# Building the decay turns on two engines: ScalarE takes four to six of eight heads, and the last batch's restacking DMAs leave from two queues

## Chip, core and metric

The kernel runs on one core of a Trainium2 chip. The metric is the device time of one execution in microseconds; lower is better. The core has TensorE (PE) for matmuls, VectorE (DVE), ScalarE (ACT) and GpSimd (POOL) for elementwise work, and SyncE (SP), which here only issues DMAs. ScalarE issues DMAs too, on a queue of its own (ACTq).

## What is computed

The input passes a linear attention with a complex decay, then a soft mixture of experts, then a feed-forward block. The change lies wholly in the first part:

```python
B, H, S, D = 4, 8, 768, 48
mag = np.sqrt(a_re * a_re + a_im * a_im)
scale = np.minimum(mag, 0.999) / (mag + 1e-06)
a_re_n, a_im_n = (a_re * scale, a_im * scale)
for t in range(S):
    ar, ai = (a_re_n[:, :, t, :, None], a_im_n[:, :, t, :, None])
    new_re = ar * S_re - ai * S_im
    new_im = ar * S_im + ai * S_re
    kv = np.einsum('bhd,bhe->bhde', k[:, :, t], v[:, :, t])
    S_re, S_im = (new_re + kv, new_im)
    y[:, :, t] = np.einsum('bhd,bhde->bhe', q[:, :, t], S_re)
...
x = _moe_ref(x=x, **moe_kwargs)      # soft routing over 8 experts x 4 slots, relu(x @ w1) @ w2
return _moe2_ref(x=x, **moe2_kwargs) # h = relu(x @ w_in); h * h @ w_out
```

## The kernel before

**Tiling.** Each of the 4 batches is cut into 6 chunks of 128 time steps, 24 chunks in all, numbered n = 0 to 23; c is a chunk's place in its batch. The recurrence becomes matmuls: running products of the decays (the scan) scale keys and queries, chunk scores are masked and applied to the values, and a state of 112x384 passes from chunk to chunk.

**Passes.** An outer loop p = 0 to 4 runs the scan of batch p beside the attention of batch p - 1. VectorE does most of the scan (`product_step`, `block_step`, `square_sums`, `turn_factors`) and, for a chunk, `key_query` (L934) and `weigh` (L916), `build_turn` (L946) and `apply_mask` (L955). The order on every engine is written out by hand; an engine stops at the first semaphore that isn't there.

**A chunk on its way.** `key_query` writes keys and queries into `xout`. SP's `stack` (L276) then moves them by 6 DMAs of 128 KB into `stk`, where a head's 48 real lanes lie on partitions 0 to 47 and its imaginary ones on 64 to 111. The turn is what multiplies the state between two chunks: for each head a 112x96 block in `stk`, a fixed 0/1 matrix `bm` times factors per row from `gst`. VectorE builds it for 8 heads in one instruction (L946), for all chunks but the last of a batch. TensorE's `scores(n)` (16 matmul instructions at L1180) waits for the six DMAs, the turn and the mask of the chunk before. ScalarE then copies the turned keys out of PSUM (`copy_kt`, two halves, L471), TensorE updates the state, ScalarE copies it (`copy_state`, L477) and the output of the chunk before (`copy_y`, L487; `copy_x`, L503; `copy_raw`, L494).

**Once per batch.** In the fifth chunk ("late") ScalarE squares the decays' products (`product_squares`, L430), VectorE sums them (L873) and makes the turns' factors `gd`, and SP's `stack_turns` (L286) moves these by 6 small DMAs into `gst`. ScalarE also writes the planes with a changed sign (`signs`, L461 to L464) without which VectorE can't start the next scan (L822).

**Fillers and weights.** `keep_busy` (L1166) puts matmuls without use between the others for the first 18 chunks; the last batch (chunks 18 to 23) has none, but for 20 ahead of `scores(18)`. The experts' weights come as halves of 768 KB, quarters of 384 KB (`load_half`, L371, and `load_part`, L377, both on ScalarE's queue) and wholes of 1536 KB (`load_w`, L291, SP).

Of the kernel before, what the change touches and what calls it, by code (L numbers as in the profile page):

```python
# [16 lines left out]
B, H, S, D = 4, 8, 768, 48  # L17
# [25 lines left out]
def program(nc, a_all, xq_all, v_all, phi, w1, w2, w_in, w_out, out):  # L43
    with ExitStack() as ctx:
        def sem(name):
            return ctx.enter_context(nc.semaphore(name))
# [150 lines left out]
        g_stacked = sem("g_stacked")  # L197
        a_done, masked, kt_copied = sem("a_done"), sem("masked"), sem("kt_copied")
        kv_done, s_copied, y_done = sem("kv_done"), sem("s_copied"), sem("y_done")
        m2_summed = sem("m2_summed")  # L200
        y_copied, x_done, x_copied = sem("y_copied"), sem("x_done"), sem("x_copied")
        last_y_copied = sem("last_y_copied")
        lgt_done, raw_copied, max_ready = sem("lgt_done"), sem("raw_copied"), sem("max_ready")
# [27 lines left out]

        def has_turn(n):
            return n % NC < NC - 1

        LOADED = [64 if k == 6 else 48 if k == 5 else 32 if k in EARLY + [10] else 16 for k in range(2 * NX)]
        ld_w = [sem(f"ld_w{k}") for k in range(2 * NX)]
# [15 lines left out]
        def _(sp):  # L252
# [16 lines left out]
            def stack(n):  # L269
                sp.wait_ge(kq_ready, 2 * (n + 1))  # L270
                if n >= NST:
                    sp.wait_ge(y_done, n - NST + 1)
                for c in range(2):
                    for t in range(DT):
                        k = c * R1 + t
                        sp.dma_start(stk[k:k + DT * (DL - 1) + 1:DT, n % NST, :, 0:2 * CH], xout[:, n % NOUT, c, t])\  # L276
                          .then_inc(stacked[n % NST], 16)

            def stack_turns(b):
                sp.wait_ge(chain, C_ALL * (b + 1))  # L280
                if b:
                    sp.wait_ge(rot_ready, (NC - 1) * b)
                for c in range(2):
                    for t in range(DT):
                        k = c * R1 + t
                        sp.dma_start(gst[k:k + DT * (DL - 1) + 1:DT],  # L286
                                     gd[:, c, t].rearrange("p c g -> p (c g)")).then_inc(g_stacked, 16)
# [77 lines left out]
        def _(act):  # L365

            def load_half(i):

                k, half = EARLY[i // 2], slice(i % 2 * KM * FE // 2, (i % 2 + 1) * KM * FE // 2)
                src = (w2 if k % 2 else w1)[k // 2].rearrange("p a b -> p (a b)")  # L370
                act.dma_start(wt[k][:, half], src[:, half]).then_inc(ld_w[k], 16)  # L371

            def load_part(k, i, j):
# [2 lines left out]
                src = (w2 if k % 2 else w1)[k // 2].rearrange("p a b -> p (a b)")  # L376
                act.dma_start(wt[k][:, part], src[:, part]).then_inc(ld_w[k], 16)  # L377

            def take_squares(b, t):
                act.wait_ge(ld_raw[t], 16 * (b + 1))  # L380
                if b == 0:

                    nc.scalar.activation(grid(U_ + t * PT, [1, PT]), grid(RAW + t * PT, [1, PT]), ACT.Square).then_inc(squares, 1)
                    return
                act.wait_ge(an_ready, DT * (b - 1) + t + 1)
                nc.scalar.activation(grid(U_ + t * PT, [1, PT]), grid(RAW + t * PT, [1, PT]), ACT.Square).then_inc(squares, 1)
                nc.scalar.activation(grid(V_ + t * PT, [1, PT]), grid(RAW + PF + t * PT, [1, PT]),
                                     ACT.Square).then_inc(squares, 1)
# [77 lines left out]
            def copy_kt(n, half):  # L466
                k = turns(n)
                act.wait_ge(a_done, 2 * n + half + 1)
                if k:
                    act.wait_ge(kv_done, k)  # L470
                nc.scalar.activation(kts[:, HB * half:HB * (half + 1), :], sk_ps(half, CH, KR), ACT.Copy).then_inc(kt_copied, 1)  # L471

            def copy_state(n):
                act.wait_ge(kv_done, turns(n) + 1)
# [83 lines left out]
            for p in range(B + 1):  # L558
                for c in range(NC + 2 * (p == B)):
# [7 lines left out]
                    if p == B - 1:  # L567
                        if c == 0:
                            act.wait_ge(an_ready, DT * B)
                        load_half(c)  # L570
                    if prepares:
                        if c < 2:
                            take_squares(p + 1, c)
# [14 lines left out]
                        copy_kt(n, 0)  # L588
                    if pair is not None:
                        copy_flipped(2 * pair)  # L590
                    if p < B and late:
                        product_squares(p, 0, 1)
                    if 0 <= n < NT and has_turn(n):
                        copy_kt(n, 1)
                    if p == B and c < NC:
                        if c == 0:
                            act.wait_ge(chain, C_ALL * B)
                            act.wait_ge(kq_ready, 2 * NC * (B - 1))
                            load_part(6, 3, 4)
                        if c >= 2:  # L600
                            load_half(NC + c)

                    if p == B and c == 1:
                        load_part(10, 0, 2)
# [16 lines left out]
                    if c == NC - 1 and prepares:  # L621
                        log_sums(p, 0)
                        log_sums(p, 1)
                        table()
                        exponential(p, 0, 1)
                    if 1 <= n < NT:
                        copy_y(n - 1)
                    if c == NC - 1 and prepares:
                        signs(p + 1)
                    if c == NC - 1 and p < B:  # L630
                        exponential(p, 1, NC - 1)
                    if pair is not None:
# [139 lines left out]
        def _(dve):  # L772
# [163 lines left out]
            def build_turn(n):  # L936
                b, c = divmod(n, NC)
                if c == 0:
                    dve.wait_ge(g_stacked, 96 * (b + 1))
                if n >= NST:  # L940
                    dve.wait_ge(kv_done, turns(n - NST + 1))
                o = stk[0:KS, n % NST, :, 2 * CH:].rearrange("p h (g d) -> p h g d", g=2)
                i = bass.AP(bm, 0, [list(bm[0:KS].ap[0]), [0, H], [0, 2], [1, D]])
                g = gst[0:KS, :, 2 * c:2 * c + 2]
                g = bass.AP(gst, g.offset, [list(g.ap[0]), [2 * (NC - 1), H], [1, 2], [0, D]])
# [211 lines left out]
        def _(pe):  # L1157
# [10 lines left out]
            def scores(n):  # L1168

                turn = has_turn(n)  # L1170
                cols = SK if turn else CH
                pe.wait_ge(stacked[n % NST], 96 * (n // NST + 1))
                if turn:
                    pe.wait_ge(rot_ready, turns(n) + 1)
                for half in range(2):
                    if n:
                        pe.wait_ge(masked, 2 * (n - 1) + half + 1)
                    for h in range(HB * half, HB * (half + 1)):
                        x = stk[0:KS, n % NST, h]
# [368 lines left out]
```

## Time and profile before

| | |
|---|---|
| median of 3 runs | 613.03 us (612.97 to 613.81) |
| profiled execution | 619.11 us, span 617.4 us |
| TensorE clock granted, mean | 0.941 of full speed |
| TensorE busy | 523.8 us, 85% |
| VectorE busy | 393.0 us, 64% |
| ScalarE busy | 336.5 us, 55% |
| GpSimd busy | 138.3 us, 22% |
| the chain that ended last | PE 61%, DVE 18%, DMA 7%, ACT 6%, issue 4%, SP's queue 3% |
| batch 0 to batch 3, first scores at | 75.2, 147.2, 223.1, 294.3 us |
| last scores at; feed-forward from | 344.7 us; 394 us |

Busy time is the sum of an engine's instructions; the chain follows back from the last instruction what released it. The profile page's strip of 40 slices shows TensorE busy in tenths as 1420569995989759988899999999999999999997 and VectorE as 5899998998999898893553351499433333333322: VectorE is full up to slice 18 (some 290 us), TensorE nearly full after slice 6 except in two dips, and from slice 24 on TensorE is full to the end. All that the change touches lies between 60 and 350 us.

### The profile page before, as it was taken

How to read it: one execution, taken by the hardware profiler on the slowest of the kernel's cores; microseconds unless marked ns; L12 is line 12 of the kernel's file. 1: busy time of each engine (PE TensorE's matmuls, PEld its weight loads, DVE VectorE, ACT ScalarE, POOL GpSimd, SP SyncE). 2: the span in 40 equal slices, each digit the busy share in tenths (PEclk: the TensorE clock that was granted, in tenths of full speed). 3: DMA queues.
4: the chain of work that ended last, by engine and by line, in shares of the span. 5: the costliest groups of instructions: out<-in, count | busy, mean ns of one | idle time of the engine just before them, and what ended most of it. 6: DMA issues, size and time to landing. Idle time of an engine off the chain costs nothing.

```text
span 617.4 us, 11733 instructions
## 1 busy us (share of the span) xinstructions
PE 523.8 (85%) x4572; PEld 396.8 (64%) x4572; DVE 393.0 (64%) x651; ACT 336.5 (55%) x590; POOL 138.3 (22%) x118
## 2 busy tenths in 40 slices
PE   1420569995989759988899999999999999999997
PEld 1210247774667547766688844578888888888886
DVE  5899998998998899893553351499433333333322
ACT  6865624795558923384243412676556555565653
POOL 7000000000000000000000000166655555555553
PEclk9975779997999969997898999999999999999999
DMA  7400656547767377976787999400101001010101
GB/s 272 153 1 0 180 157 134 123 99 191 212 156 149 92 166 200 213 187 142 158 214 202 389 428 427 197 1 2 53 0 53 0 1 51 2 51 2 51 1 51
DMA packets 41607, 79.59 MB, mean 129 GB/s; under 512 B 7376, under 2 KB 29008, under 8 KB 40400
## 3 DMA queue, kind: packets, MB, share of 16 engines
q1 hardware_dynamic: 39104, 67.44, 38.6%
q10 hardware_dynamic: 2448, 11.40, 5.8%
q8 instruction: 36, 0.59, 0.4%
q14 instruction: 19, 0.16, 0.1%
HBM read 55.12 MB, written 4.72 MB: 97 GB/s over the span
## 4 chain that ended last, share of the span: by engine, by line
PE 61%; DVE 18%; DMA 7%; ACT 6%; issue 4%; SPq 3%; DVEq 0%; ACTq 0%
PE ps L1477 10%; PE ps L1473 10%; PE ps L1474 10%; PE ps L1180 8%; DMA stk<-xout 5%; PE ps L1166 3%; PE ps L1447 3%; SPq L276 3%; DVE tt L838 3%; DVE big L844 2%; DVE tt L840 2%; PE ps L1223 2%; PE ps L1220 2%; DVE xout L934 2%; PE ps L1367 2%
## 5 line engine op out<-in xcount | busy, mean ns | idle before, releaser
L1145 DVE TENSOR_TENSOR qs<-rs 128x512 f32<-128x512 f32 x96 | 82.7, 862 | 118.8 <-ACT rs L707 118.8
L768 POOL TENSOR_TENSOR hlo<-qs,hhi 128x512 fp32r<-128x512 f32 x96 | 126.1, 1314 | 125.4 <-DVE qs L1145 120.2
L1180 PE MATMUL ps<-stk 112*128 112x224 f32 (+1 forms) x384 | 87.0, 388 | 29.7 <-DMA stk<-xout 29.7
L1473 PE MATMUL ps<-hhi,who 128*128 128x512 f32 x285 | 111.0, 389 | 0.0
L1474 PE MATMUL ps<-hhi,wlo 128*128 128x512 f32 x285 | 110.9, 389 | 0.0
L1180 PEld LDWEIGHTS ps<-stk 112*128 112x128 f32 x384 | 76.8, 218 | 42.0 <-DMA stk<-xout 33.7
L707 ACT ACTIVATE rs<-ps 128x512 f32<-128x512 f32 x96 | 57.4, 598 | 82.2 <-PE ps L1447 82.1
L1166 PE MATMUL ps<-ident 128*32 128x512 bf16 x256 | 71.6, 396 | 32.0 <-DVE xout L934 32.0
L1477 PE MATMUL ps<-hlo,who 128*128 128x512 f32 x285 | 80.5, 391 | 0.1
L760 POOL MEMSET sinz<- 128x768 f32 x1 | 0.7, 738 | 337.9 <-PE ps L1223 337.9
L711 ACT ACTIVATE hhi<-rs 128x512 fp32r<-128x512 f32 x96 | 60.8, 633 | 3.1
L1477 PEld LDWEIGHTS ps<-hlo,who 128*128 128x128 f32 x285 | 53.2, 188 | 12.1 <-POOL hlo L768 1.3
L1473 PEld LDWEIGHTS ps<-hhi,who 128*128 128x128 f32 x285 | 53.5, 188 | 11.2
L1474 PEld LDWEIGHTS ps<-hhi,wlo 128*128 128x128 f32 x285 | 53.5, 188 | 11.1
L1166 PEld LDWEIGHTS ps<-ident 128*32 128x32 bf16 x256 | 20.8, 98 | 55.0 <-issue 41.7
L471 ACT ACTIVATE kts<-ps 128x384 f32<-128x384 f32 x40 | 19.3, 486 | 61.6 <-PE ps L1180 61.6
L955 DVE TENSOR_TENSOR asb<-ps,mask 128x512 f32<-128x512 f32 x48 | 32.7, 687 | 30.8 <-ACT kts L471 24.3
L934 DVE TENSOR_TENSOR xout<-big,xq 128x768 f32<-128x768 f32 x48 | 45.8, 953 | 0.5
L1447 PE MATMUL ps<-cst,ust 128*128 128x512 f32 x96 | 37.4, 392 | 0.2 <-DVE ust L1127 0.2
L1223 PE MATMUL ps<-asb,vr 128*48 128x128 f32 x384 | 35.4, 272 | 0.0
L1220 PE MATMUL ps<-stk,st 112*48 112x128 f32 x320 | 31.8, 276 | 0.0
L1242 PE MATMUL ps<-xts,phs 112*32 112x128 f32 x576 | 26.4, 281 | 4.3 <-issue 4.1
(161 smaller groups left out, 809.5 us busy)
## 6 DMA issues: line engine op xcount, KB each, us to landing
stk<-xout SPq DMA_DIRECT2D x144, 128.0 KB, 3.9
wt<-in_w SPq DMA_DIRECT2D x8, 1536.0 KB, 16.8
big<-in_a_all SPq DMA_DIRECT2D x12, 768.0 KB, 5.6
xq<-in_xq SPq DMA_DIRECT2D x24, 384.0 KB, 4.6
wt<-in_w ACTq DMA_DIRECT2D x12, 768.0 KB, 5.8
vr<-in_v_all SPq DMA_DIRECT2D x24, 192.0 KB, 4.4
out<-ost SPq DMA_DIRECT2D x5, 768.0 KB, 3.5
wins<-in_w_in SPq DMA_DIRECT2D x1, 3072.0 KB, 23.1
```

The costliest lines, as they stand in the source:

```text
L707: nc.scalar.activation(rs[:, i % NQS, :], ps[:, i % 2, :], ACT.Relu).then_inc(relu_ready, 1)
L711: nc.scalar.activation(hhi[:, i % NHS, :], rs[:, i % NQS, :], ACT.Square).then_inc(hi_ready, 1)
L768: pool.tensor_tensor(hlo[:, i % NHS, :], qs[:, i % NQS, :], hhi[:, i % NHS, :].bitcast(F32), ALU.subtract).then_inc(lo_ready, 1)
L934: dve.tensor_tensor(o, e, x, ALU.mult).then_inc(kq_ready, 1)
L1145: dve.tensor_tensor(qs[:, i % NQS, :], rs[:, i % NQS, :], rs[:, i % NQS, :], ALU.mult).then_inc(sq_ready, 1)
L1166: nc.tensor.matmul(ps[P - SL:P, bank, :], idb[:, 0:SL], idle, start=True, stop=True)
L1180: last = nc.tensor.matmul(ps[:, h // 2, h % 2 * SK:h % 2 * SK + cols], x[:, 0:CH], x[:, CH:CH + cols], start=True, stop=True)
L1223: last = nc.tensor.matmul(y, vr[:, n % NV, h * D:(h + 1) * D], asb[:, n % 2, h], start=(c == 0), stop=True)
L1447: nc.tensor.matmul(ps[:, i % 2, :], ust[:, f * P:(f + 1) * P], cst[:, t * TW:(t + 1) * TW], start=True, stop=True).then_inc(g_done, 1)
L1473: nc.tensor.matmul(accs[k], wh[k], hi, start=(f == 0), stop=False)
L1474: nc.tensor.matmul(accs[k], wl[k], hi, start=False, stop=False)
L1477: last = nc.tensor.matmul(accs[k], wh[k], lo, start=False, stop=(f == F2B - 1))
```

## The change

1. **Turns.** `act_heads(n)` says how many of the 8 heads ScalarE builds: 4 for c = 1 to 3 of batches 0 and 1, 6 for c = 1 to 4 of batch 2, none for c = 0 or in batch 3. ScalarE makes two copies of 112x48 per head, each with a scale per row; half of a turn's copies stand behind `copy_kt(n - 1, 1)`, half behind `copy_y(n - 2)`. VectorE's instruction covers the other heads.
2. **Late chunk.** `copy_kt(n, 1)` now stands ahead of the second `product_squares`.
3. **Early signs.** In a batch's last chunk `signs` stands ahead of `copy_y`, not behind it.
4. **Two queues.** In batch 3 SP issues three of a chunk's six restacking DMAs, and three of `stack_turns`; ScalarE issues the rest: `stack(18)` at the batch's start, `stack(n + 1)` behind `copy_kt(n, 1)`.
5. **Weights.** `load_half` 2 to 5 go one chunk earlier; `load_part(6, 3, 4)` moves from chunk 18 to 19.

```diff
+        def act_heads(n):
+            b, c = divmod(n, NC)
+            return 0 if c == 0 or b == B - 1 or not has_turn(n) else 6 if b == B - 2 else 4 if c < 4 else 0
...
-                for c in range(2):
+                for c in range(1 if n >= NT - NC else 2):
                     for t in range(DT):
                         k = c * R1 + t
                         sp.dma_start(stk[k:k + DT * (DL - 1) + 1:DT, n % NST, :, 0:2 * CH], xout[:, n % NOUT, c, t])\
...
+            def stack(n):
+                act.wait_ge(kq_ready, 2 * (n + 1))
+                act.wait_ge(y_done, n - NST + 1)
+                for t in range(DT):
+                    k = R1 + t
+                    act.dma_start(stk[k:k + DT * (DL - 1) + 1:DT, n % NST, :, 0:2 * CH], xout[:, n % NOUT, 1, t])\
+                       .then_inc(stacked[n % NST], 16)
...
+            def build_turn(n, part):
+                b, c = divmod(n, NC)
+                count = act_heads(n) // 2
+                if count == 0:
+                    return
+                act.wait_ge(g_stacked, 96 * (b + 1))
+                if n >= NST:
+                    act.wait_ge(kv_done, turns(n - NST + 1))
+                for h in range(H - (2 - part) * count, H - (1 - part) * count):
+                    for g in range(2):
+                        o = 2 * CH + g * D
+                        last = nc.scalar.activation(stk[0:KS, n % NST, h, o:o + D], bm[0:KS, :], ACT.Copy,
+                                                    scale=gst[0:KS, h, 2 * c + g:2 * c + g + 1])
+                if part:
+                    last.then_inc(rot_act, 1)
...
-                        load_half(c)
+                        for i in ((0,), (1, 2), (3,), (4,), (5,), ())[c]:
+                            load_half(i)
+                    if p == B and c == 0:
+                        stack(n)
...
+                    if 0 <= n < NT and has_turn(n):
+                        copy_kt(n, 1)
+                    if 0 <= n < NT - 1:
+                        build_turn(n + 1, 0)
                     if p < B and late:
                         product_squares(p, 0, 1)
-                    if 0 <= n < NT and has_turn(n):
-                        copy_kt(n, 1)
...
+                    if p == B and c < NC - 1:
+                        stack(n + 1)
...
+                        signs(p + 1)
+                    if p == B - 1 and c == NC - 1:
+                        stack_turns(p)
                     if 1 <= n < NT:
                         copy_y(n - 1)
-                    if c == NC - 1 and prepares:
-                        signs(p + 1)
+                    if 0 <= n < NT - 1:
+                        build_turn(n + 1, 1)
...
+                heads = H - act_heads(n)
+                o = stk[0:KS, n % NST, 0:heads, 2 * CH:].rearrange("p h (g d) -> p h g d", g=2)
...
+                    if act_heads(n):
+                        pe.wait_ge(rot_act, act_turns(n))
```

ScalarE's order in the late chunk of batch 0 (n = 4) up to the table load; `kts` is `copy_kt`, `chain` the count of VectorE's scan. Before:

```order
L430 ACTIVATE big<-big 128x6x288 [waits chain]
L471 ACTIVATE kts<-ps 128x384 [waits kv_done,a_done]
L525 ACTIVATE lgx<-ps 128x2x32 [waits flipped]
L430 ACTIVATE big<-big 128x6x288 [waits chain]
L471 ACTIVATE kts<-ps 128x384 [waits kv_done,a_done]
L430 ACTIVATE big<-big 128x6x96 [waits chain] x2
```

With the change:

```order
L458 ACTIVATE big<-big 128x6x288 [waits chain]
L499 ACTIVATE kts<-ps 128x384 [waits kv_done,a_done]
L570 ACTIVATE lgx<-ps 128x2x32 [waits flipped]
L499 ACTIVATE kts<-ps 128x384 [waits kv_done,a_done]
L458 ACTIVATE big<-big 128x6x288 [waits chain]
L458 ACTIVATE big<-big 128x6x96 [waits chain] x2
```

The second key copy and the second large square pass have changed places.

ScalarE's order in chunk 20 of the last batch, from its key copies to the state's copy. Before:

```order
L471 ACTIVATE kts<-ps 128x384 [waits kv_done,a_done]
L525 ACTIVATE lgx<-ps 128x2x32 [waits sums_done,flipped]
L471 ACTIVATE kts<-ps 128x384 [waits kv_done,a_done]
L371 DMA wt_76<-in_w 128x1536
L487 ACTIVATE xts<-ps 128x512 [waits x_done,y_done]
L525 ACTIVATE lgx<-ps 128x2x32 [waits sums_done,flipped]
L477 ACTIVATE st<-ps 112x384 [waits y_done,kv_done]
```

With the change:

```order
L499 ACTIVATE kts<-ps 128x384 [waits kv_done,a_done]
L570 ACTIVATE lgx<-ps 128x2x32 [waits sums_done,flipped]
L499 ACTIVATE kts<-ps 128x384 [waits kv_done,a_done]
L396 DMA stk<-xout 16x8x256 [waits y_done,kq_ready]
L396 DMA stk<-xout 16x8x256 x2
L382 DMA wt_76<-in_w 128x1536
L532 ACTIVATE xts<-ps 128x512 [waits x_done,y_done]
```

Three restacking DMAs of chunk 21 now stand behind the second key copy of chunk 20 and ahead of `copy_y(19)`.

SP's order behind the last chunk but one, with the change:

```order
L286 DMA stk<-xout 16x8x256 [waits y_done,kq_ready]
L286 DMA stk<-xout 16x8x256 x2
L302 DMA wt_83<-in_w 128x3072 [waits kq_ready]
L308 DMA wt_80<-in_w 128x768
L302 DMA wt_82<-in_w 128x3072
L308 DMA wt_85<-in_w 128x1536 [waits stacked2]
```

Before, five DMAs instead of two followed the first: 3.4 MB of weights now stand three DMAs closer to SP's `stack(23)`, while the other half of that stack leaves from ScalarE.

## Rows read from the trace of the kernel before

**Rows 1.** Busy time of each engine in two stretches: batch 0's middle; chunks 19 and 20
```profile
88.00:133.00 45.00, 44.31 (x597) 33.74 (x597) 40.74 (x74) 29.02 (x51) 0.00 (x0) 0.93 0.60 142
...
305.00:325.00 20.00, 18.45 (x272) 15.72 (x272) 9.51 (x13) 7.29 (x18) 0.00 (x0) 0.91 0.95 212
```

**Rows 2.** Timeline of PE, scores of chunks 6, 8, 12, 18 to 21 and 23
```profile
147.22 5.60 PE L1180 MATMUL ps<-stk 112*128 112x224 f32 x16 [6.48 <-DMA stk<-xout]
...
171.66 3.29 PE L1180 MATMUL ps<-stk 112*128 112x224 f32 x16 [1.77 <-DMA stk<-xout]
...
223.12 5.19 PE L1180 MATMUL ps<-stk 112*128 112x224 f32 x16 [9.64 <-DMA stk<-xout]
...
294.26 3.29 PE L1180 MATMUL ps<-stk 112*128 112x224 f32 x16
...
305.21 4.98 PE L1180 MATMUL ps<-stk 112*128 112x224 f32 x16 [1.86 <-DMA stk<-xout]
314.28 3.29 PE L1180 MATMUL ps<-stk 112*128 112x224 f32 x16
325.35 4.98 PE L1180 MATMUL ps<-stk 112*128 112x224 f32 x16 [1.58 <-DMA stk<-xout]
...
344.72 2.05 PE L1180 MATMUL ps<-stk 112*128 112x128 f32 x16
```

**Rows 3.** Timeline of DVE: where it stands idle (idle us and releaser in brackets)
```profile
142.37 0.18 DVE L822 COPY a<-big 128x36 f32<-128x36 f32 x1 [1.77 <-ACT big L464]
...
200.61 0.69 DVE L955 TENSOR_TENSOR asb<-ps,mask 128x512 f32<-128x512 f32 x1 [1.32 <-ACT kts L471]
...
290.41 0.96 DVE L946 TENSOR_TENSOR stk<-bm,gst 112x768 f32<-112x768 f32 x1 [10.02 <-DMA gst<-gd]
```

**Rows 4.** Groups by line and form, 60 to 352 us: busy us, mean ns of one
```profile
L946 DVE TENSOR_TENSOR stk<-bm,gst 112x768 f32<-112x768 f32 x20 | 19.0, 952 | 10.0 <-DMA gst<-gd 10.0
L916 DVE TENSOR_TENSOR xq<-xq,big 128x384 f32<-128x384 f32 x24 | 13.2, 552 | 0.5 <-ACT big L449 0.5
L509 ACT ACTIVATE eb<-eb 32x256 f32<-32x256 f32 x11 | 5.5, 499 | 2.6 <-DVE eb L961 2.4
...
L517 ACT ACTIVATE scale_diag<-sel,rescale 96x32 f32<-96x32 f32 x10 | 3.2, 321 | 0.3
```

**Rows 5.** Timeline of ACT: batch ends, a late chunk, key copy of chunk 20
```profile
137.60 0.60 ACT L487 ACTIVATE xts<-ps 128x512 f32<-128x512 f32 x1 [0.67 <-PE ps L1223]
138.09 0.52 ACT L461 ACTIVATE big<-big 128x384 f32<-128x384 f32 x1
...
198.51 1.64 ACT L430 ACTIVATE big<-big 128x1728 f32<-128x1728 f32 x1
200.05 0.47 ACT L471 ACTIVATE kts<-ps 128x384 f32<-128x384 f32 x1
...
290.76 0.27 ACT L494 ACTIVATE eb<-ps 96x128 f32<-96x128 f32 x1
...
317.94 0.48 ACT L471 ACTIVATE kts<-ps 128x384 f32<-128x384 f32 x1
```

**Rows 6.** The chain that ended last: start, us, what
```profile
215.80 7.28 DMA stk<-xout
...
280.70 9.69 DMA gst<-gd
```

**Rows 7.** Queues of ACT and SP: start of issue, us for all, count
```profile
214.75 0.34 ACTq L371 DMA_DIRECT2D wt<-in_w  x1
...
321.56 17.16 SPq L276 DMA_DIRECT2D stk<-xout  x12
338.76 0.60 SPq L291 DMA_DIRECT2D wt<-in_w  x1
```

**Rows 8.** DMA landing: the tile `gst`, and the page's group of stk<-xout
```profile
DMA to landing us min/median/max: 1.8/1.8/9.7
...
stk<-xout SPq DMA_DIRECT2D x144, 128.0 KB, 3.9
```

More of the change, by code:

```diff
@@ L199, in program @@
         kv_done, s_copied, y_done = sem("kv_done"), sem("s_copied"), sem("y_done")
-        m2_summed = sem("m2_summed")
+        m2_summed, rot_act = sem("m2_summed"), sem("rot_act")
         y_copied, x_done, x_copied = sem("y_copied"), sem("x_done"), sem("x_copied")
@@ L233, in has_turn, with act_turns @@
             return n % NC < NC - 1
+        def act_heads(n):
+            b, c = divmod(n, NC)
+            return 0 if c == 0 or b == B - 1 or not has_turn(n) else 6 if b == B - 2 else 4 if c < 4 else 0
+        def act_turns(n):
+            return sum(act_heads(k) > 0 for k in range(n + 1))
         LOADED = [64 if k == 6 else 48 if k == 5 else 32 if k in EARLY + [10] else 16 for k in range(2 * NX)]
@@ L282, in stack_turns @@
                     sp.wait_ge(rot_ready, (NC - 1) * b)
-                for c in range(2):
+                    sp.wait_ge(rot_act, act_turns(NC * b - 1))
+                for c in range(1 if b == B - 1 else 2):
                     for t in range(DT):
@@ L377, in load_part, with stack_turns @@
                 act.dma_start(wt[k][:, part], src[:, part]).then_inc(ld_w[k], 16)
+            def stack(n):
[5 more added lines that the diff above has]
+                       .then_inc(stacked[n % NST], 16)
+            def stack_turns(b):
+                act.wait_ge(chain, C_ALL * (b + 1))
+                act.wait_ge(rot_ready, (NC - 1) * b)
+                act.wait_ge(rot_act, act_turns(NC * b - 1))
+                for t in range(DT):
+                    k = R1 + t
+                    act.dma_start(gst[k:k + DT * (DL - 1) + 1:DT], gd[:, 1, t].rearrange("p c g -> p (c g)")).then_inc(g_stacked, 16)
             def take_squares(b, t):
@@ L590, in _ @@
                         copy_flipped(2 * pair)
+                    if 0 <= n < NT and has_turn(n):
+                        copy_kt(n, 1)
+                    if 0 <= n < NT - 1:
+                        build_turn(n + 1, 0)
                     if p < B and late:
                         product_squares(p, 0, 1)
-                    if 0 <= n < NT and has_turn(n):
-                        copy_kt(n, 1)
[L595 to L601, printed above, removed]
+                    if p == B and c < NC - 1:
+                        stack(n + 1)
+                    if p == B and c == 1:
+                        act.wait_ge(chain, C_ALL * B)
+                        act.wait_ge(kq_ready, 2 * NC * (B - 1))
+                        load_part(6, 3, 4)
+                    if p == B and 2 <= c < NC:
+                        load_half(NC + c)
                     if p == B and c == 1:
@@ L941, in build_turn @@
                     dve.wait_ge(kv_done, turns(n - NST + 1))
-                o = stk[0:KS, n % NST, :, 2 * CH:].rearrange("p h (g d) -> p h g d", g=2)
-                i = bass.AP(bm, 0, [list(bm[0:KS].ap[0]), [0, H], [0, 2], [1, D]])
+                heads = H - act_heads(n)
+                o = stk[0:KS, n % NST, 0:heads, 2 * CH:].rearrange("p h (g d) -> p h g d", g=2)
+                i = bass.AP(bm, 0, [list(bm[0:KS].ap[0]), [0, heads], [0, 2], [1, D]])
                 g = gst[0:KS, :, 2 * c:2 * c + 2]
-                g = bass.AP(gst, g.offset, [list(g.ap[0]), [2 * (NC - 1), H], [1, 2], [0, D]])
+                g = bass.AP(gst, g.offset, [list(g.ap[0]), [2 * (NC - 1), heads], [1, 2], [0, D]])
                 dve.tensor_tensor(o, i, g, ALU.mult).then_inc(rot_ready, 1)
```

## The prediction, made before the changed kernel was run

> **What bounds the kernel now.** I read the busy times by stretch first. From 88 to 133 us TensorE is busy 44.3 of 45.0 us: there a chunk costs what TensorE's own list costs, fillers included, and time saved on VectorE buys nothing. In chunks 19 and 20 the DMA engines are 95% taken [rows 1]. Then the scores on TensorE's timeline, since every chunk starts with them. Where they waited, they waited for the restacked keys: 6.48 us at chunk 6, 1.77 at chunk 8, 9.64 at chunk 12, 1.86 at 19, 1.58 at 21 [rows 2]. Those waits are VectorE's lateness (it makes the keys) plus the DMAs' time. VectorE itself is full in these stretches and stood idle for three releasers that the change touches: the sign planes (1.77 us), ScalarE's second key copy (1.32), the turn factors' DMA (10.02) [rows 3]. The last batch takes 344.72 - 294.26 = 50.46 us for five steps. Everything behind it (experts, feed-forward) is not edited and moves as a block.
>
> **The change part by part.** All sums are against the profiled execution (619.11 us; span 617.4); the median of the three runs is 613.03, 6.1 us less, and I take the difference over unchanged. About 0.2%, 1.2 us, is what a measurement of this kernel can tell from no change.
>
> *Smaller turns on VectorE.* 8 heads (768 columns) take 952 ns, and 384 columns of a like instruction 552 ns [rows 4], so a column costs 1.04 ns. Four heads fewer save 0.40 us (six turns), six fewer 0.60 us (four turns): 4.8 us of VectorE in all. In batch 0 and the middle of batch 2 TensorE sets the pace: nothing. In batch 1 turns 7 and 8 stand ahead of the keys of chunks 8 and 9, which were late: 0.8 us by chunk 9.
>
> *The copies on ScalarE.* 6 x 8 + 4 x 12 = 96 copies of 48 columns with a scale per row. The trace has no such form. With a per-row operand, 32 columns take 321 ns and 256 take 499 [rows 4]: 334 ns for 48. ScalarE's starts follow each other 0.11 us sooner than a duration (137.60 + 0.60 against 138.09) [rows 5], so 0.23 us each; 22 us in all. Bounds: 0.21 (as 32 columns) and 0.39 (as 256). Their cover is ScalarE's waits for TensorE ahead of `copy_y` and `copy_state`: it is busy 29.0 of 45.0 us there [rows 1], so 3.7 us a chunk are idle for 1.9 us of copies. It is thin in chunks 1 and 7, where squares stand there too: I charge 0.35 us in batch 0 and 0.7 in batch 1, with 0 and 3 as bounds over all. Per head VectorE pays 0.10 us and ScalarE 0.46. The Trainium skill ("ScalarE: Activation LUTs", Rules for kernel authors) says to multiply on VectorE, not ScalarE. By that rule alone the trade of 4.8 us for 22 would lose; by the idle time it costs about 1.
>
> *Second key copy first.* In the late chunk the large square pass (1.54 us from start to start) stood ahead of it [rows 5]. VectorE waited 1.32 us for the copy [rows 3], masked for 0.69 and only then summed the squares. Now the mask is done while the pass ends, and the sums start with its end: 0.6 us, in batches 0 and 1. In batch 2 the mask stands behind the sums, which get the pass 0.4 us later: -0.4 of the gain there.
>
> *Early signs.* They stood behind `copy_y`, which waited 0.67 us and took 0.49 [rows 5]; VectorE waited 1.77 us for the last of them [rows 3]. Ahead of it they end 1.2 us sooner, in batches 1 and 2. Price: `copy_y` comes behind 4.2 us of signs, 3.8 us later than before in batch 1 and 2.0 in batch 2, and TensorE's transposes with it. The waits of 6.48 and 9.64 us that follow [rows 2] hide that.
>
> So at chunk 6: 0.6 - 0.35 = 0.3 us earlier. VectorE's next scan: 0.9 (it then waits 1.2 us, not 1.77). Chunk 9: 0.9 + 0.8, less a little of ScalarE's copies, is 1.6. The keys of chunk 12: 1.6 + 0.6 = 2.2.
>
> *Chunk 12.* Its last restacking DMA took 7.28 us to land [rows 6] against a median of 3.9 [rows 8]: half 0 of the weights left at 214.75 [rows 7], in the middle of the six. That half stands behind `copy_raw(10)`, hence behind logits that wait for the delayed `copy_y`. So it leaves near 214.6 still, while the six leave 2.2 us sooner and should land in about 4.5: 2.8 more. Chunk 12 is 5.0 us earlier (bounds 2.2 and 7.0, the latter with the clock kept up, below). In batch 2 VectorE is only 2.8 us ahead, 3.4 after the turn of 13, and chunk 14 waits for it a little: 4.5 are left, and 4.1 at chunk 17.
>
> *Turn factors of batch 3.* The last of six DMAs of 5 KB took 9.69 us [rows 6], where the common one takes 1.8 [rows 8], with half 5 of the weights issued half a microsecond behind it. Half 5 now goes a chunk earlier. ScalarE's three leave only behind the logits of chunk 15, near 277.5, and should land near 281, not 290.4. This takes 9 us from VectorE's wait of 10.02; but chunk 18 was ready at 294.26 only through TensorE's own list (20 fillers), so it frees no more than the lateness of chunk 19 (1.86).
>
> *Two queues.* SP needs 3.8 us for six issues, over 0.6 each (twelve took 17 us with a wait between) [rows 7]. Half of that is saved only if ScalarE's three leave as early. They don't: they stand behind `copy_kt(n - 1, 1)`, 3.68 us after the scores' start (317.94 against 314.28) [rows 2, 5], though the keys were long ready. Scores to scores is then 3.68 + 2 x 0.64 + 3.9 = 8.9 us at least. TensorE's own list needs about 9.3 us in even chunks and 7.4 to 8.3 in odd ones (9.07 from 305.21, less 1.7 for the slow start). For chunk 18 they stand behind `copy_raw(16)`, at 290.76 [rows 5] less 4.1: with 1.28 for the issues and 3.9 they land at 291.8, or some 0.5 sooner, as an issue leaves while an earlier copy still runs; TensorE would be ready at 290.2. So chunk 18 starts near 291.4, 2.8 us earlier than before. For chunk 23 they meet the weights: SP's 3.4 MB (from 338.76 [rows 7]) leave 2 us closer to its keys and ahead of ScalarE's three. The nearest row is the small DMA caught by a half: 9.69 us. I take 7 to land, so 12 us for that step; bounds 9.4 and 13. Sum of the five steps: 9.2 + 9.2 + 9.9 + 9.6 + 12 = 49.9, against 50.46: 0.5 earlier. The clock (below) is as likely to cost 0.6 once more as not, and I take the two as even.
>
> Forecast: 2.8 us earlier at the end of the attention: 613.0 - 2.8 = **610.2 us**.
>
> **The rivals.**
>
> *A. The clock stays up.* Chunks 6, 12, 19 and 21 take 5 us or more for scores that take 3.29 elsewhere; chunk 8 doesn't, after 1.77 us idle [rows 2]. The long ones fall in stretches at the lower level (1.2 of 2.4 GHz). With the late transposes TensorE is idle 6.48 - 3.8 - 0.3 = 2.4 us ahead of chunk 6 and 9.64 - 2.0 - 5.0 = 2.6 ahead of 12. If the clock holds, each gives 1.8 us, 19 another 1.7: with the 2.8 some 8 us, **605**. Against it: after 1.58 and 1.86 us idle it fell.
>
> *B. ScalarE's queue sets the last batch's pace: slower.* If its three land in 6.3 us, as under weights, not 3.9, each of five steps is 3.68 + 1.28 + 6.3 = 11.3 us; five are 56.3, 5.8 more than before, chunk 18 loses 2.4 of its 2.8: 613.0 - 0.4 + 5.8 = 618.4; with two of the five so, 615. It decides from a landing of 5.1 us on, where a step costs the 10.1 of before. For it: DMA is 95% taken [rows 1], and idle TensorE lowers the clock, which delays the key copy by 1.3. Against: the weights stand behind the three on the same queue. The skill ("DMA: Bandwidth & Descriptors", Queues, rings and completion order) says that a completion lands only after all earlier writes of that DMA engine, across queues, so splitting does not shield a stack from SP's 3.4 MB. The 9.69 us row agrees. The same page (Issuing engines are not separate DMA queues) allows a second queue nothing but the issue time.
>
> *C. Given back.* The gains of batches 1 and 2 come, but chunk 12's keys still take 7.3 us to land: 2.2 us are left there, 0.9 behind chunk 18's wait, and a last step of 13 us makes the five 50.9 and takes 0.4 more: 0.5 left, **612.5**, no change. It decides if half 0 leaves as early as the stack does.
>
> **How the numbers follow.** Forecast 0.46, its range 608 to 611.5; A 0.22; B 0.16; C 0.16. Faster by over 0.2% (below 611.8): the forecast, A and a little of C, 0.69. Within 0.2%: 0.16. Slower: 0.15. For 8 in 10 the range runs from A, 604.5, to two bad steps of B, 615.
>
> **What would show it.** Right: scores of 12 near 218 after a landing of 4 to 5 us; VectorE's wait for the signs near 1.2; turn factors landed near 281; ACT copies of 0.33 us; steps of 9 to 10 us in the last batch with waits of 0 to 2 on restacking DMAs, and the longest before 23. Wrong: a gap ahead of chunk 8 or 12 as before, TensorE waiting for `rot_act`, ScalarE's `copy_state` late in batch 2, or a last batch over 52 us.

## The result, and the profile after

The changed kernel takes **629.88 us** (median of 6 runs, 624.09 to 631.25) against 613.42 for the kernel before beside it: a ratio of 1.0249 [1.0201, 1.0298]. The prediction was 610.2 us, faster; its range ended at 615. The profiled execution is an ordinary one (629.77 us, span 628.0). Ratios, here and below, stand with their 95% intervals and leave out the few runs that fell in a slower state of the chip; the medians keep them.

Timeline of PE of the changed kernel, the scores of chunks 6, 8, 12, 14, 18, 22 and 23 (start us, us, instruction, in brackets the idle time before it and its releaser), as [rows 2]:

```profile
145.97 5.04 PE L1237 MATMUL ps<-stk 112*128 112x224 f32 x16 [1.12 <-DMA stk<-xout]
...
172.91 3.54 PE L1237 MATMUL ps<-stk 112*128 112x224 f32 x16
...
220.54 5.30 PE L1237 MATMUL ps<-stk 112*128 112x224 f32 x16 [0.55 <-DMA stk<-xout]
...
247.09 4.97 PE L1237 MATMUL ps<-stk 112*128 112x224 f32 x16 [3.83 <-DMA stk<-xout]
...
297.99 3.29 PE L1237 MATMUL ps<-stk 112*128 112x224 f32 x16 [1.00 <-DMA stk<-xout]
...
334.72 3.29 PE L1237 MATMUL ps<-stk 112*128 112x224 f32 x16
...
354.03 3.78 PE L1237 MATMUL ps<-stk 112*128 112x128 f32 x16 [8.82 <-DMA stk<-xout]
```

Chunk 12 is 2.6 us earlier than in [rows 2] (223.12); by chunk 18 that is lost (297.99 against 294.26); and chunk 23 starts 19.31 us after chunk 22, where the kernel before took 9.42 (344.72 in [rows 2] less the start of chunk 22):

```profile
335.30 3.29 PE L1180 MATMUL ps<-stk 112*128 112x224 f32 x16
```

TensorE stands idle for 8.82 us for one DMA. The chain of waits of the changed kernel names it in its last row (the first is a wait for chunk 14's stack, taken up at the end), and the answer for `stk<-xout` on ScalarE's queue gives the landing:

```profile
238.36 8.69 DMA stk<-xout
...
339.00 1.19 ACTq L396
340.23 13.76 DMA stk<-xout
```
```profile
DMA to landing us min/median/max: 2.7/3.5/13.8
```

The queues of the changed kernel at that place (start of issue, us for all, count), as [rows 7]:

```profile
331.31 0.61 ACTq L382 DMA_DIRECT2D wt<-in_w  x1
331.95 0.48 ACTq L388 DMA_DIRECT2D wt<-in_w  x1
338.40 2.45 ACTq L396 DMA_DIRECT2D stk<-xout  x3
...
334.91 0.62 SPq L302 DMA_DIRECT2D wt<-in_w  x1
335.57 0.59 SPq L308 DMA_DIRECT2D wt<-in_w  x1
336.20 0.78 SPq L302 DMA_DIRECT2D wt<-in_w  x1
354.00 0.33 SPq L308 DMA_DIRECT2D wt<-in_w  x1
```

SP has done its own half of stack 23 and issues 3.4 MB of weights from 334.91 on; ScalarE's half follows from 338.40 and lands at 353.99. SP's own half, issued 0.7 to 1.9 us ahead of the weights, took 6.9 to 7.9 us to land; ScalarE's three took 8.9, 12.9 and 13.8. From 340 to 354 us the DMA engines are full:

```profile
340.00:354.00 14.00, 5.03 (x102) 3.14 (x99) 0.42 (x1) 3.36 (x9) 0.00 (x0) 0.77 1.01 330
```

The last three numbers are TensorE's granted clock (0.77), the DMA engines' busy share (all of it) and 330 GB/s.

The turns and the signs stand in the trace as priced (groups by form; timeline of DVE, as [rows 3]):

```profile
L513 ACT ACTIVATE stk<-bm,gst 112x48 f32<-112x48 f32 x96 | 23.5, 325 | 0.0
...
L1001 DVE TENSOR_TENSOR stk<-bm,gst 112x384 f32<-112x384 f32 x6 | 3.3, 553 | 0.0
L1001 DVE TENSOR_TENSOR stk<-bm,gst 112x192 f32<-112x192 f32 x4 | 1.4, 352 | 0.0
```
```profile
139.80 0.18 DVE L876 COPY a<-big 128x36 f32<-128x36 f32 x1 [1.16 <-ACT big L492]
...
214.93 0.18 DVE L876 COPY a<-big 128x36 f32<-128x36 f32 x1 [1.27 <-ACT big L492]
...
290.49 0.96 DVE L1001 TENSOR_TENSOR stk<-bm,gst 112x768 f32<-112x768 f32 x1 [6.02 <-DMA gst<-gd]
```

The copies take 325 ns (334 expected) and 23.5 us in all (22), the turns 553 and 352 ns, and VectorE waits 1.2 us for the signs instead of 1.8. VectorE's busy time falls from 393.0 to 388.2 us, the 4.8 us of the sum.

The two first profiles differ by 10.7 us and the medians by 16.5, since the profiled execution of before was 6 us above its own median. The first experiment asks where those 6 us lay.

### The profile page after: what moved, and what is told of

It reads as the page before. It is cut to its first block, busy times and chain, and to the rows that moved or that the text cites. A ratio compares the mean times of both kernels' runs of the same rounds, so it can differ in the third digit from the quotient of the medians.

```text
span 628.0 us, 11862 instructions
## 1 busy us (share of the span) xinstructions
PE 528.5 (84%) x4572; PEld 397.0 (63%) x4572; DVE 388.2 (62%) x651; ACT 357.1 (57%) x686; POOL 138.2 (22%) x118
## 4 chain that ended last, share of the span: by engine, by line
PE 60%; DVE 14%; ACT 10%; DMA 8%; issue 4%; SPq 2%; ACTq 1%; DVEq 0%
PE ps L1534 10%; PE ps L1530 10%; PE ps L1531 10%; PE ps L1237 8%; DMA stk<-xout 6%; PE ps L1221 3%; PE ps L1504 3%; DMA big<-in_a_all 3%; DVE tt L892 2%; DVE big L898 2%; DVE tt L894 2%; PE ps L1299 2%; SPq L286 2%; PE ps L1277 2%; PE ps L1424 2%
## 5 line engine op out<-in xcount | busy, mean ns | idle before, releaser
L1237 PE MATMUL ps<-stk 112*128 112x224 f32 (+1 forms) x384 | 83.5, 377 | 24.0 <-DMA stk<-xout 24.0
L1221 PE MATMUL ps<-ident 128*32 128x512 bf16 x256 | 75.9, 415 | 31.4 <-DVE xout L988 31.4
L1237 PEld LDWEIGHTS ps<-stk 112*128 112x128 f32 x384 | 74.1, 212 | 36.2 <-DMA stk<-xout 28.5
L1534 PEld LDWEIGHTS ps<-hlo,who 128*128 128x128 f32 x285 | 53.2, 188 | 12.1 <-POOL hlo L822 1.4
L1299 PE MATMUL ps<-xts,phs 112*32 112x128 f32 x576 | 28.7, 297 | 5.5 <-issue 5.5
## 6 DMA issues: line engine op xcount, KB each, us to landing
wins<-in_w_in SPq DMA_DIRECT2D x1, 3072.0 KB, 16.8
```

What stands on the lines that cost most here:

```text
L1221: nc.tensor.matmul(ps[P - SL:P, bank, :], idb[:, 0:SL], idle, start=True, stop=True)
L1534: last = nc.tensor.matmul(accs[k], wh[k], lo, start=False, stop=(f == F2B - 1))
```

## The experiments

"Step 22 to 23" is from the scores of chunk 22 to those of 23, in each run's own profile. All ratios are to the kernel before, run beside it on the same chip. Its median there was 611.3 to 613.4 us, so medians of different rows can be compared to some 2 us only. Each chunk's start is from one execution. In short:

| kernel | median us | ratio | chunk 12 at | 18 at | 18 to 22 | 22 to 23 |
|---|---|---|---|---|---|---|
| before, profile shown ahead | 613.03 | 1 | 223.1 | 294.3 | 41.0 | 9.4 |
| before again | 613.41 | 1.0013 [0.9985, 1.0040] | 221.8 | 293.1 | 34.6 | 9.4 |
| the change | 629.88 | 1.0249 [1.0201, 1.0298] | 220.5 | 298.0 | 36.7 | 19.3 |
| its stack 23 on SP | 616.88 | 1.0057 [1.0016, 1.0098] | 217.4 | 294.8 | 36.2 | 9.8 |
| its last batch on one queue | 612.33 | 0.9963 [0.9924, 1.0002] | 217.3 | 294.3 | 34.4 | 9.4 |
| its SP weights held back | 621.61 | 1.0141 [1.0076, 1.0206] | 216.3 | 295.9 | 37.2 | 9.9 |
| one queue, old halves | 608.75 | 0.9960 [0.9944, 0.9976] | 217.2 | 288.2 | 35.8 | 9.4 |
| key order and signs | 609.48 | 0.9971 [0.9948, 0.9995] | 217.9 | 288.8 | 37.7 | 9.4 |
| two queues alone | 628.66 | 1.0278 [1.0241, 1.0315] | 222.4 | 294.5 | 39.4 | 20.1 |
| turns alone | 612.82 | 1.0021 [1.0001, 1.0040] | 223.4 | 293.5 | 39.4 | 9.4 |
| two queues, issued early | 620.24 | 1.0120 [1.0090, 1.0150] | 221.2 | 293.3 | 34.4 | 17.1 |
| signs alone | 608.75 | 0.9942 [0.9914, 0.9969] | 216.5 | 286.4 | 40.5 | 9.4 |
| key order alone | 612.03 | 1.0003 [0.9978, 1.0029] | 221.7 | 293.2 | 37.3 | 9.4 |
| change, old halves, early issue | 618.41 | 1.0095 [1.0071, 1.0120] | 217.9 | 289.3 | 35.0 | 17.9 |
| stack 23 alone on two queues | 623.34 | 1.0179 [1.0139, 1.0218] | 223.4 | 294.8 | 34.2 | 17.9 |
| signs, five stacks early | 609.25 | 0.9953 [0.9925, 0.9980] | 221.7 | 293.8 | 34.5 | 9.4 |

### The kernel before again

> The kernel before, unchanged, for a second profiled execution. The first one took 619.11 us where the median of its runs is 613.4, so the two profiles differ by 10.7 us and the medians by 16.5. If the first profiled execution was an unlucky one, a new one takes 612 to 615 us, and its chunks must start earlier somewhere by 4 to 7 us in all: the place of that difference is what the comparison of the two first profiles cannot show. If profiling itself costs the kernel before 5 us, the new one takes 618 to 620 again. Timed, it must be within 0.2% of the kernel before (ratio 0.998 to 1.002); what it differs is the noise of all that follows.

Measured: 611.31 us profiled, so the first profiled execution was the unlucky one. Its chunks 18 and 23 on the timeline of PE:

```profile
293.06 3.10 PE L1180 MATMUL ps<-stk 112*128 112x224 f32 x15
...
327.64 3.29 PE L1180 MATMUL ps<-stk 112*128 112x224 f32 x16
337.06 2.05 PE L1180 MATMUL ps<-stk 112*128 112x128 f32 x16
```

Chunk 18 starts 1.2 us earlier than in [rows 2], chunk 23 7.7 us earlier: the last batch's five steps take 44.0 us, not 50.46. The waits of 1.86 and 1.58 us at chunks 19 and 21 and the low clock behind them were that execution's. VectorE's wait for the turn factors is 5.99 us here, not 10.02, and it ends at 286.3, 4.2 us sooner than in the change: the 6.02 of the change shows no gain. Over the kernels with one queue in the table, 18 to 22 takes 34.2 to 41.0 us; this stretch falls out differently from execution to execution.

### Stack 23: another queue, or the bulk beside it?

```diff
-                for c in range(1 if n >= NT - NC else 2):
+                for c in range(1 if NT - NC <= n < NT - 1 else 2):
...
-                    if p == B and c < NC - 1:
+                    if p == B and c < NC - 2:
                         stack(n + 1)
```
(SP also waits for the stacks of all three buffers ahead of `load_part(10, 2, 4)`.)

> The change, but all six transfers of the last key stack, that of chunk 23, are on SP's queue, ahead of SP's 3.4 MB of weights; ScalarE keeps its halves of chunks 18 to 22 and of the turn factors. Theory T1 (SP's bulk takes the DMA engines from a small stack on the other queue), T2 (ScalarE's own bulk stands ahead of it in its queue) and T3 (ScalarE only issues it late, behind a key copy) all expect the landing to go back from 13.8 us to 4 to 6 us, the scores of chunk 23 to start near 345 us instead of 354.0, and 629.9 less 8 to 9.5 us, so 620.5 to 622. If the stack is not what costs, the time stays within 2 us of 629.9.

Measured: 616.88 us, below the 620.5 to 622 expected, and step 9.8: stack 23 is worth 13.0 us of the change by the medians, 1.9% or 11.8 us by the ratios. Three theories had one expectation here; the next run parts them. It moves SP's wait for stack 23 ahead of `load_w(8)`, and leaves ScalarE as it is in the change.

> The change, with SP's 3.4 MB of weights (three transfers issued at 334.9 to 337.0 us) held back until the stack of chunk 23 has landed; ScalarE's queue is as in the change. T1 (SP's bulk takes the DMA engines): ScalarE's half of stack 23 lands 4 to 7 us after its issue at 340.2, the scores of chunk 23 start at 345 to 347, and the time falls by 6 to 9 us to 621 to 624, unless the weights that come later cost some of it again. T2 (ScalarE's own 1.15 to 1.5 MB ahead of it in its queue): the landing stays at 11 to 14 us and the time at 628 to 632 or above. T3 (late issue alone): landing 4 us after the issue in neither, since the issue at 340.2 is not moved; it is already out of favour, as 13.8 us lie behind the issue.

Measured: 621.61 us, step 9.9. The line of `stk<-xout` on ScalarE's queue in that stretch, then its queue, which still had 1.15 MB of weights ahead of the three:

```profile
DMA to landing us min/median/max: 3.7/3.8/4.5
```
```profile
329.70 0.61 ACTq L382 DMA_DIRECT2D wt<-in_w  x1
330.34 0.47 ACTq L388 DMA_DIRECT2D wt<-in_w  x1
336.79 1.88 ACTq L396 DMA_DIRECT2D stk<-xout  x3
```

The same three transfers, issued as in the change, land in 3.7 to 4.5 us instead of 13.8 when SP's bulk isn't there. T1 stands. T2 falls, since ScalarE's own weights were ahead of the three as before, and T3, since they still stood behind the key copy. The weights held back cost 5.1 us more than the second profile of before behind chunk 23 (620.6 - 343.01 = 277.6 against 609.6 - 337.06 = 272.5), so this is no mend.

### One queue; and each part alone

"One queue" takes back `range(1 if ...)` in both SP helpers and ScalarE's calls of `stack` and `stack_turns`.

> The change without its last part: all restacks and the turn factors of the last batch are on SP's queue again; turns on ScalarE, order of the key copies, early signs and the early half load stay. From the profiles: the steps of chunks 18 to 23 go back from 36.3 us (18 to 22) plus 19.3 (22 to 23) to 41.0 plus 9.4, so 5.2 us less, and the turn factors land 3 to 4 us later: 629.9 - 5.2 + 3.5 = 628.2 us, if two queues were worth what my prediction said in chunks 18 to 22. If the other parts of the change were neutral it would be at 613, like the kernel before; so what it lies above 613.4 is what turns, order, signs and the early half load cost together. I expect 624 to 629.

Measured: 612.33 us, ratio 0.9963: the rest of the change costs nothing. The expected 624 was built on the first profile's 41.0 us, and missed. The run with stack 23 on SP lies 4.5 us above it by the medians and 0.9%, 5.7 us, by the ratios: that is what the late halves of chunks 18 to 22 and of the turn factors cost (1.8 us of it between 18 and 22, by the two profiles). Its chunk 14 waited:

```profile
243.07 4.98 PE L1231 MATMUL ps<-stk 112*128 112x224 f32 x16 [1.96 <-DMA stk<-xout]
```

The next run undoes the pair of half loads at chunk 13 as well:

```diff
-                        for i in ((0,), (1, 2), (3,), (4,), (5,), ())[c]:
-                            load_half(i)
+                        load_half(c)
```

> The kernel of the run with one queue, and besides the six half loads of batch 3's weights go out one per chunk again, as in the kernel before, instead of two together at chunk 13. Theory T4: the two halves issued together (230.7 us there, 1.5 MB) share the DMA engines with stack 14, whose transfers then end 2.0 us after TensorE is ready, and TensorE's clock is lower for the scores of chunk 14 (4.98 us instead of 3.29); so the steps 13 to 14 and 14 to 15 fall from 11.65 and 12.83 to the 9.6 and 11.15 of the kernel before, 3.7 us in all, and the time to about 609 (median of the one queue run 612.3). Rival: the collision is with something else and the steps stay; then 612. Against the kernel before it should then be 0.3 to 0.8% faster.

Measured: 608.75 us. Chunk 14 starts 9.62 us after 13 (11.65 with the pair), without a wait, and 15 follows after 11.15 (12.83): T4's 3.7 us are in the profile. In time the medians differ by 3.6 us but the ratios don't (0.9960, 0.9963); the run with the pair scattered from 605.6 to 619.0 us, this one from 607.2 to 611.2. So the pair's cost in time is not settled. In the profiles it is plain: from chunk 13 to 15 the four kernels with the pair took 24.5 to 28.0 us, the other twelve profiles 20.8 to 21.5.

> The same as the last, and besides ScalarE makes no turns: VectorE makes all of them. What is left of the change is the second key copy ahead of the product squares and the early signs. If the turns on ScalarE were worth the 0.8 us that my prediction gave them (and cost ScalarE 1.05), it is within 1 us of the last one. If the gain at chunk 12 (217 us against 222 to 223) is the turns' and not the signs', the scores of chunk 12 start at 221 or later and the time is 3 to 4 us above the last one.

Measured (`act_heads` returns 0): 609.48 us, 0.7 us above the last. Chunk 12 starts at 217.9 us: the signs and the key order bring it forward; the turns don't.

> The kernel before with the last part of the change alone: batch 3's restacks and turn factors on two queues, ScalarE's halves behind its first key copies. (One quarter load moves from chunk 18 to 19 as in the change.) T1: stack 23 lands 10 to 14 us after its issue beside SP's 3.4 MB, and the time is 11 to 17 us above the kernel before, 623 to 628. From the second profile of the kernel before, its steps from chunk 18 to chunk 22 take 34.6 us; two queues give 36.2 in the runs so far, so there is no gain to set against that. If the stack of 23 is late only because of what the other parts do, the time stays within 4 us of the kernel before.

Measured: 628.66 us, the whole loss of the change from its last part alone. On ScalarE's line the landing is again

```profile
DMA to landing us min/median/max: 2.8/3.9/14.5
```

and step 22 to 23 takes 20.1 us. The time is 0.7 us over the 623 to 628 expected. Against the second profile of before (18.6 us of span), 1.4 us are lost by chunk 18, 4.8 from 18 to 22, 10.7 in the last step and 1.7 behind it.

> The kernel before with the turns of 4 to 6 heads on ScalarE alone: old order of the key copies, signs at their old place, one queue, one half load per chunk. (One quarter load moves from chunk 18 to 19.) By my prediction it is worth 0.8 us less 1.05 us, so within 1 us of the kernel before; by the rival that turns also free ScalarE's place in no way, it is slower by up to 2 us. If it is faster by 3 us or more, the turns and not the signs make the gain by chunk 12.

Measured: 612.82 us, ratio 1.0021 [1.0001, 1.0040]: nothing, or up to 0.4% lost.

> The kernel before with the early signs alone. My prediction charged chunk 12 with most of 5 us from them; the run with signs and key order together is 0.3% faster (609.5 against 611.4) and starts the scores of chunk 12 at 217.9 instead of 221.8 us. If the signs carry that, chunk 12 starts at 218 to 219 here and the time is 609.5 to 610.5; if the key order carries it, 221.5 and 611.4.

Measured: 608.75 us, ratio 0.9942, as good as any kernel here. Queues of SP around chunk 12 in the second profile of before, then with signs alone:

```profile
212.03 3.88 SPq L276 DMA_DIRECT2D stk<-xout  x6
```
```profile
209.16 5.07 SPq L276 DMA_DIRECT2D stk<-xout  x6
```

The six leave 2.9 us sooner and are down by 216.5; ScalarE's half load leaves at 214.07 against 214.29.

> The kernel before with the second key copy ahead of the product squares alone. The other side of the last run: by my prediction 0.6 us by chunks 6 and 12 and 0.4 us against it in batch 2, so within 0.2% of the kernel before; if it, not the signs, brings chunk 12 forward, 609.5 to 610.

Measured: 612.03 us, ratio 1.0003: nothing, on either side.

### Would an earlier issue on ScalarE do?

```diff
+                    if p == B and c < NC - 1:
+                        stack(n + 1)
                     if 0 <= n < NT and has_turn(n):
                         copy_kt(n, 0)
```
(and the call behind the key copies goes), on the kernel with two queues alone.

> The kernel before with two queues for batch 3's restacks (the run that took 628.7 us), and ScalarE now issues its half of the next chunk's stack ahead of its first key copy instead of behind it. Theory T5 (order): ScalarE's half is late because it is issued behind a copy that waits for the scores (298.2 us there, where VectorE had written the rotated keys at 302.1 less the next chunk's lead; on one queue all six are out by then), and the last one, issued at 337.5, falls behind the 3.4 MB that SP had issued at 334.0 to 335.8. Then it is now issued near 332, before SP's bulk, lands in 4 to 6 us, and the time falls by 10 to 17 us to 612 to 618. T1 in its strict form (any small stack on the second queue is slow beside bulk, in whatever order): the landing stays above 9 us and the time at 622 or above. For both: if two queues are then any good, the steps 18 to 22 take less than the 34.6 us of one queue; my guess is 34 to 36.

Measured: 620.24 us, so 8.4 us less by the medians and 9.7 by the ratios, and neither theory as written. Chunks 18 to 22 are back at 34.4 us: there it was the order (T5). One profile could not tell, as one queue alone gave 34.2 to 41.0 us; but the four profiles with the late order on two queues took 36.2 to 39.4, and the three with the early one, this and two below, 34.4 to 35.0. But for stack 23 the issue starts at 328.76, 0.36 us behind SP's first weights, and the third transfer still takes 13.9 us:

```profile
328.40 0.59 SPq L302 DMA_DIRECT2D wt<-in_w  x1
```
```profile
328.76 2.81 ACTq L396 DMA_DIRECT2D stk<-xout  x3
```

So this run did not test what T5 expected, an issue ahead of the bulk from the other queue; no run here did.

The same order in the whole change (with the old halves):

> The whole change with one half load per chunk as before, and ScalarE's stack halves issued ahead of its first key copy. By T5: the parts up to chunk 17 give what they gave on one queue (608.75), and two queues in batch 3 cost nothing or up to 3 us: 608 to 613. If early issue makes two queues as good as I had predicted (0.5 us and more a chunk), 604 to 607. By strict T1: 620 or above.

Measured: 618.41 us, between its cases: step 22 to 23 takes 17.9 us, the rest is as on one queue.

### The last stack alone, and the five others alone

> The kernel before, with ScalarE issuing three transfers only: its half of the stack of chunk 23, behind its first key copy. All else of the last batch, the turn factors too, is on SP. (One quarter load moves from chunk 18 to 19.) If the collision of this one small stack with SP's 3.4 MB is the main cost, the step 22 to 23 takes 17 to 20 us and the time is 8 to 11 us above the kernel before, 620 to 623; the rest of the 17 us of the run with two queues alone (628.7) is then the lateness of chunks 18 to 22. If the five other halves must be late too for the last to be, it is within 3 us of the kernel before.

Measured: 623.34 us, 12.1 above the kernel before beside it (8 to 11 expected), with three transfers of 128 KB moved to the other queue. TensorE waits 7.89 us for them:

```profile
346.87 3.78 PE L1233 MATMUL ps<-stk 112*128 112x128 f32 x16 [7.89 <-DMA stk<-xout]
```

Two queues alone cost 17.3 us above the kernel before beside them; the last stack is 12.1 of it, and the other 5.2 fit the 4.5 to 5.7 that the two runs above gave for the late halves.

> The early signs alone (608.75 us), and besides ScalarE's halves of chunks 18 to 22 and of the turn factors on its own queue, issued ahead of its first key copy, with the stack of chunk 23 wholly on SP. If two queues are worth anything when nothing is issued late and no bulk is beside, the time is 606 to 608. If the restacks of the last batch are hidden behind TensorE on one queue already (34.6 us of 18 to 22 in the second profile of the kernel before, 34.4 with early issue), it is 608 to 610.

Measured: 609.25 us against 608.75 for signs alone: two queues give nothing in chunks 18 to 22 even with an early issue and stack 23 on SP. The turn factors were not free of weights, though: in this profile ScalarE issued half 5 at 280.83, 0.45 us ahead of its three, the slowest took 6.0 us to land, and VectorE waited 9.1 us. In this profile also chunk 12 came late in spite of the early signs, as rival C described it:

```profile
211.55 5.11 SPq L286 DMA_DIRECT2D stk<-xout  x6
```
```profile
214.74 6.90 DMA stk<-xout
```

## Why the prediction was wrong

**The step that failed** is *Two queues*: "The nearest row is the small DMA caught by a half: 9.69 us. I take 7 to land, so 12 us for that step; bounds 9.4 and 13." It landed in 13.76 us and the step took 19.31. The row was the nearest in kind, not in size: 0.77 MB stood beside it, here it was 3.4 MB on the other queue. In five runs the whole stack was down only when the bulk was, however long it had itself been out. The table has the landing of SP's last 1536 KB, the start of the scores of chunk 23, the time from SP's first weight to those scores, and the lag of ScalarE's first issue behind that weight:

| kernel | bulk down at us | scores at us | bulk to scores us | lag us |
|---|---|---|---|---|
| two queues, issued early | 344.6 | 344.82 | 16.4 | 0.4 |
| change, early issue | 342.0 | 342.20 | 17.2 | 0.4 |
| stack 23 alone | 346.5 | 346.87 | 17.3 | 3.1 |
| the change | 353.5 | 354.03 | 19.1 | 3.5 |
| two queues alone | 353.5 | 353.93 | 20.0 | 3.5 |

For the change the landing of SP's two wholes of 1536 KB (issued at 334.91 and 336.20; the second took the 17.3) reads:

```profile
DMA to landing us min/median/max: 11.5/14.4/17.3
```

The page of before held the right row: its weights on SP took 16.8 us to land.

```profile
wt<-in_w SPq DMA_DIRECT2D x8, 1536.0 KB, 16.8
```

Laid beside the changed kernel's issue at 334.9 it gives 351.7, and a last step of 17.

By the runs, then: 613.4 us before, 17.3 more for the two queues, 2.4 less for signs, key order and turns make 628.3; the 1.6 us left are within what these runs tell apart, and the pair of halves may be in them.

Rival B named this collision. But B was priced at a landing of 6.3 us in every step, not at the bulk's own time in one, so its 618.4 was 11.5 us short of 629.9, and it got 0.16. The Trainium skill ("DMA: Bandwidth & Descriptors", Queues, rings and completion order) says that a completion lands only after all earlier writes of its DMA engine, across queues. The last of the three transfers fits it: it lands 0.2 to 0.5 us behind the bulk in all five runs. The first does not wait for all that was issued before it: in the change it was down at 347.3, 6.2 us ahead of a whole that SP had issued 2.2 us sooner. So the order of issue is not the order of writes, and how the engines share two queues is not shown here.

**The term's other side failed too.** The 50.46 us of the last batch, from which "9.2 + 9.2 + 9.9 + 9.6 + 12" should gain 0.5, were the longest of what this batch takes: on one queue 43.8 to 50.5 us in the profiles here, and 44.0 in the second profile of before. I had written that the profiled execution lay 6.1 us above the median and "take the difference over unchanged"; those 6 us lay in the very stretch on which the sum rested. The five earlier halves, issued "behind `copy_kt(n - 1, 1)`", were read rightly as late, but set against those 50 us they looked free; they cost 4.5 to 5.7. (Their 3.68 us is 3.66 by the rows, 317.94 less 314.28, which changes nothing.) The Trainium skill's rule on the same page (Issuing engines are not separate DMA queues), that a second queue saves only the issue time, agrees with the last run: it saved nothing.

**Right:** the parts ahead of the last batch. The forecast gave them 2.8 us at chunk 18; everything but the last batch's edits and the pair of halves measures 0.4%, 2.4 us. That the two are so close is in part luck: in the profiles of the three one-queue kernels with early signs and no pair, chunk 18 started 4.3 to 6.7 us sooner than in the second profile of before, and the last batch gave 1.2 to 5.9 us of it back. Chunk 12 was to start near 218: it did at 216.3 to 217.9 in seven of the eight kernels above with early signs (221.7 in the eighth), and at 220.5 in the change itself, whose chunk 8 came 3 to 5 us later than in the four kernels closest to it. The last restacking DMA of chunk 12 landed in 4.5 us there, as forecast, not in 7.28. Ahead of chunk 8 ScalarE stood 3.20 us for a DMA that took 10.11 us:

```profile
156.10 10.11 DMA big<-in_a_all
```

That is the "gap ahead of 8" named as a sign of failure. The turns on ScalarE seem to have a part in it: four of the seven profiles with them show this wait at 1.95 to 4.14 us, the longest with turns alone, whose chunk 8 starts at 172.91 too; none of the nine without them is over 1.26. Why three of the seven don't have it is open. **Second key copy:** 0.6 us expected, nothing measurable. **Turns:** a gain of 0.8 us against a cost of 1.05 expected, 0 to 0.4% slower measured. **Signs:** nearly all of the gain. **Turn factors** "should land near 281": they were only issued at 285.41 and landed at 290.5. **Half 5 a chunk earlier** did help them: their slowest transfer landed in 3.0 to 3.9 us in the four kernels that have it, and in 5.2 to 9.8 us in eleven of the twelve profiles that don't. But moving the halves up makes a pair of halves 1 and 2 at chunk 13, and the pair is what chunk 14 waited for, a collision that I hadn't looked for. **Given back:** against the second profile of before the change led by 1.3 us at chunk 12 and was 4.9 behind at 18; 5.6 of these 6.2 us were lost between chunks 13 and 15, where the pair of halves goes out and stack 14 took 8.69 us to land.

The best versions are the early signs alone (0.9942) and everything of the change but the two queues and the pair (0.9960), which can't be told apart.

## What to carry to other kernels

Before a small transfer on which an engine waits moves to another queue, add up what all queues will have out at that moment, and take the landing of that bulk as its price. On the bulk's own queue, ahead of it, these transfers landed in 3.2 to 8.8 us in fifteen profiles. If the profiled execution is far from the median, find the stretch in which it is, and don't book gains there. Test a rearrangement in several parts one part at a time: here one edit gained 0.6% and another lost 2.8%.

## What the runs showed of the hardware that was not expected

- A small lag behind a bulk on the other queue is as bad as a large one: three transfers of 128 KB, the first issued 0.4 us behind the first of 3.4 MB, took up to 13.9 us, about as long as those issued 3.5 us behind (13.8). Without the bulk they took 3.7 to 4.5. What an issue ahead of the bulk from the other queue would do, no run shows.
- One and the same kernel spent 44.0 and 50.5 us on its last attention batch in two profiled executions, through two waits under 2 us for a landing, each followed by scores at the lower clock (4.98 us instead of 3.29).
